# Gram stage with eight chunk places, tile-wise first loads on two queues, unread matmuls ahead of it, and another order of vector work around the first quad

## The reference

```python
# q, k, v: (1, 6016, 256); w_in: (256, 2048), w_out: (2048, 256), twice
qn = q / (np.linalg.norm(q, axis=1, keepdims=True) + 1e-06)   # norm over the 6016 tokens
kn = k / (np.linalg.norm(k, axis=1, keepdims=True) + 1e-06)
s = kn.transpose(0, 2, 1) @ qn / tau                          # 256 x 256
s = s - s.max(-1, keepdims=True)
a = np.exp(s); a /= a.sum(-1, keepdims=True) + 1e-09
x = v @ a
h = x @ w_in1;  r = np.maximum(h, 0.0);  x = (r * r) @ w_out1
h = x @ w_in2;  y = np.maximum(0.01 * h, h) @ w_out2
```

## Time and profile before

| | |
|---|---|
| median of 3 runs | 1044.88 us |
| the profiled execution | 1044.72 us, its span 1042.9 us (1.8 us lie around the span) |
| PE busy | 1025.2 us, 98% |
| DVE busy | 733.9 us, 70% |
| ACT busy | 670.3 us, 64% |
| granted TensorE clock, mean | 0.999 of full |
| DMA moved | 69.24 MB |

### The profile page before, as it was taken

The page is one execution under the profiler, slowest core; times in us unless marked ns, Lnnn a source line. Parts: engine busy times, 40 slices in busy tenths (PEclk is TensorE's granted clock), DMA queues, the critical chain, the costliest instruction groups (busy, mean ns, idle before and its releaser), DMA issues.

```text
span 1042.9 us, 13073 instructions
## 1 busy us (share of the span) xinstructions
PE 1025.2 (98%) x4596; PEld 858.9 (82%) x4596; DVE 733.9 (70%) x1176; ACT 670.3 (64%) x1155; POOL 0.8 (0%) x7
## 2 busy tenths in 40 slices
PE   7989999999999999999999999999999999999998
PEld 6868888888888888888888888888888888888886
DVE  6888866657666665766657777777777777767665
ACT  5768877767767777667676655556556555555553
POOL 0000000000000000000000000000000000000000
PEclk9999999999999999999999999999999999999999
DMA  8810111122122112205344002002002002000001
GB/s 297 317 60 21 31 50 71 66 96 70 47 94 84 53 56 100 76 29 189 120 166 155 1 1 80 1 1 79 1 1 79 0 1 80 1 1 26 14 1 41
DMA packets 33552, 69.24 MB, mean 66 GB/s; under 512 B 2768, under 2 KB 18128, under 8 KB 33488
## 3 DMA queue, kind: packets, MB, share of 16 engines
q1 hardware_dynamic: 33488, 68.43, 19.3%
HBM read 44.56 MB, written 23.86 MB: 66 GB/s over the span
## 4 chain that ended last, share of the span: by engine, by line
PE 93%; DVE 3%; DMA 1%; ACT 1%; issue 1%; SPq 0%; ACTq 0%; DVEq 0%
PE bank L443 30%; PE bank L445 30%; PE bank L444 30%; PE bank L450 2%; DMA qk<-in_k 1%; DVE sq_sum L877 1%; DVE xop_lo L911 0%; DVE raw L902 0%; DVE g L1077 0%; ACT park_down L719 0%; ACT g L770 0%; DVE wi_lo L883 0%; ACT qk_hi L640 0%; DVE qk_lo L871 0%; DVE sq_sum L887 0%
## 5 line engine op out<-in xcount | busy, mean ns | idle before, releaser
L738 ACT ACTIVATE g_hi<-g 128x496 fp32r<-128x496 f32 (+1 forms) x384 | 237.2, 618 | 214.3 <-DVE g L1031 76.4
L1021 DVE TENSOR_TENSOR g_lo<-g,g_hi 128x496 fp32r<-128x496 f32 (+1 forms) x384 | 259.9, 677 | 128.7 <-ACT g_hi L738 127.1
L445 PE MATMUL bank<-g_hi,wout_lo 128*128 128x496 f32 (+1 forms) x768 | 296.4, 386 | 0.0
L444 PE MATMUL bank<-g_lo,wout_hi 128*128 128x496 f32 (+1 forms) x768 | 296.0, 385 | 0.0
L443 PE MATMUL bank<-g_hi,wout_hi 128*128 128x496 f32 (+1 forms) x768 | 295.9, 385 | 0.0
L443 PE MATMUL bank<-xop_hi,win_hi 128*128 128x496 f32 (+1 forms) x672 | 260.2, 387 | 4.1 <-DVE win_lo L936 2.2
L444 PE MATMUL bank<-xop_lo,win_hi 128*128 128x496 f32 (+1 forms) x672 | 259.3, 386 | 0.0
L445 PE MATMUL bank<-xop_hi,win_lo 128*128 128x496 f32 (+1 forms) x672 | 259.0, 385 | 0.0
L443 PEld LDWEIGHTS bank<-g_hi,wout_hi 128*128 128x128 f32 x768 | 144.3, 188 | 27.5
L444 PEld LDWEIGHTS bank<-g_lo,wout_hi 128*128 128x128 f32 x768 | 144.3, 188 | 27.3
L445 PEld LDWEIGHTS bank<-g_hi,wout_lo 128*128 128x128 f32 x768 | 144.2, 188 | 27.0
(11 more groups left out here) (98 smaller groups left out, 665.8 us busy)
## 6 DMA issues: line engine op xcount, KB each, us to landing
up_parts<-park_up SPq DMA_DIRECT2D x8, 896.0 KB, 4.3
qk<-in_q SPq DMA_DIRECT2D x15, 384.0 KB, 4.6
qk<-in_k SPq DMA_DIRECT2D x15, 384.0 KB, 6.2
stage_o<-in_w_out SPq DMA_DIRECT2D x16, 256.0 KB, 3.4
down_parts<-park_down SPq DMA_DIRECT2D x8, 512.0 KB, 2.8
raw<-in_vT SPq DMA_DIRECT2D x8, 496.0 KB, 4.9
x_tiles<-out_buf SPq DMA_DIRECT2D x8, 496.0 KB, 2.8
raw<-x_tiles SPq DMA_DIRECT2D x8, 496.0 KB, 4.2
```

Source lines behind the costliest of these rows:

```text
L444: pe.matmul(out, a_hi, b_lo, start=False, stop=False, **more)
L445: last = pe.matmul(out, a_lo, b_hi, start=False, stop=stop and i == len(operands) - 1, **more)
L738: act.activation(g_hi[:, tile, 0:W], g[:, tile, 0:W], ACT.Copy).then_inc(g_hi_made[tile], 1)
L1021: dve.tensor_tensor(g_lo[:, tile, 0:W], g[:, tile, 0:W], g_hi[:, tile, 0:W].bitcast(F32), ALU.subtract).then_inc(g_split[tile], 1)
```

## The change

Loads: the Gram stage has eight chunk places, the loops are written out, and the first edge tile comes alone (128 KB each of q and k). Its k and the k of chunks 0 and 1 are issued from ACT's queue, the rest from SP's. The second edge tile comes ahead of chunk 3, raw0 behind the second piece of w_in1. PE does seven matmuls on a constant tile ahead of the first load; nobody reads them. The sums stand behind the first tile of the last chunk instead of ahead of it. Around the first quad the order of ACT, DVE and PE work is another, and DVE's `fold_scale_first` goes to ACT.

```diff
-QK_SLOTS = 5
+QK_SLOTS = 8
-SPLIT_SLOTS = (2,)
+SPLIT_CHUNKS = (2, 7, 12)
+EARLY_CHUNKS = 2
+WARM_UP = 7
...
+            def load_chunk(c):
+                if c >= QK_SLOTS:
+                    sp.wait_ge(chunk_used, c - QK_SLOTS + 1)
+                    sp.wait_ge(squared, squares_at(c - QK_SLOTS) + 1)
...
+            sp.dma_start(edge[:, 0, 0, :], q_t[:, 0, :]).then_inc(edge_loaded[0], 16)
+            for c in range(EARLY_CHUNKS):
+                sp.dma_start(qk[:, c, 0, :, :], q_t[:, chunk_tokens(c), :]).then_inc(qk_loaded[c], 16)
+            for c in range(EARLY_CHUNKS, QK_CHUNKS):
+                if c == EDGES_AFTER:
+                    load_edge(1)
+                load_chunk(c)
...
-                if c == 2 * QK_SLOTS - 1:
-                    load_raw0()
...
                 sp.dma_start(held, w_in1_b[:, :, n * FCOLS:(n + 1) * FCOLS]).then_inc(stage_loaded[n], 16)
+                if n == 1:
+                    load_raw0()
...
+            pe.wait_ge(constants, 1)
+            for i in range(WARM_UP):
+                pe.matmul(fold[0][:, 0:P], ones[:, :], ones[:, :], start=True, stop=True)
...
+                    if c == QK_CHUNKS - 1 and t == 0:
+                        pe.wait_ge(chunk_added, QK_CHUNKS + 1 + QK_TILES)
+                        for i in range(2):
+                            for b in range(CB):
+                                total = pe.matmul(sums[:, i, b, :], sq_sum[:, i, 0, b * P:(b + 1) * P], ones[:, 0:2],
+                                                  start=True, stop=True)
+                        total.then_inc(sums_ready, 1)
...
                 product(0, bank_a[:, 0:W], A11, B11, True).then_inc(p1_ready, 1)
-                fold_unit(4)
...
                 product(0, bank_c[:, 0:W], S1, T1, True).then_inc(p5_ready, 1)
-                fold_unit(5)
+                fold_unit(4)
...
                 product(0, bank_a[:, 0:W], A12, B21, False).then_inc(c11_ready, 1)
+                fold_unit(5)
                 fold_unit(6)
...
+            act.dma_start(edge[:, 1, 0, :], k_t[:, 0, :]).then_inc(edge_loaded[0], 16)
+            for c in range(EARLY_CHUNKS):
+                act.dma_start(qk[:, c, 1, :, :], k_t[:, bass.ds(EDGES + c * QK_TILES, QK_TILES), :]
+                              ).then_inc(qk_loaded[c], 16)
...
-            x_high(0, 0)
             weights_hi(0)
             weights_hi(1)
...
             act.activation(warm[:, 1:2], ones[:, 0:1], ACT.Exp)
+            x_high(0, 0)
             x_high(0, 1)
             weights_hi(2)
...
-                x_high(0, 2)
-                x_high(0, 3)
                 fold_scale(0, 0)
+                fold_scale(0, 1)
                 up_high(0)
...
             x_sum(0, T1)
-            weights_lo(0)
...
-            weights_lo(1)
+            weights_lo(0)
             dve.wait_ge(q_row_ready, 1)
...
+                if Q == 0:
+                    up_sums_low(1)
                 if G == 0:
                     down_low(quad)
-                if Q == 0:
-                    up_sums_low(1)
```

More of the change, by code:

```diff
@@ L151, in channel_attention_two_mlps @@
         qk = at("qk", [P, QK_SLOTS, 2, QK_TILES, C], F32, o_xh0)
[L152 to L156, removed]
+        sq_sum = at("sq_sum", [P, 2, QK_TILES, C], F32, o_xh0 + 49152)
+        edge = at("edge", [P, 2, EDGES, C], F32, o_xh0 + 55296)
+        qk_hi = at("qk_hi", [P, 2, QK_TILES, C], F32R, o_wout_hi)
+        qk_lo = at("qk_lo", [P, 2, QK_TILES, C], F32R, o_wout_hi + 6144)
         sq = at("sq", [P, SQ_SLOTS, 2, QK_TILES, C], F32, o_wout_hi + 12288)
@@ L187, in channel_attention_two_mlps @@
         assert UNITS == len(fold)
-        edge_loaded = sem("edge_loaded")
+        edge_loaded = [sem(f"edge_loaded{t}") for t in range(EDGES)]
         qk_loaded = [sem(f"qk_loaded{i}") for i in range(QK_SLOTS)]
@@ L277, in chunks_before, with squares_at @@
         def chunks_before(part, low):
-            last_byte = (7 * low + part + 1) * ROW_COLS * 4 - 1
-            return QK_CHUNKS - QK_SLOTS + min(last_byte // SLOT_BYTES, QK_SLOTS - 1) + 1
+            slot = ((7 * low + part + 1) * ROW_COLS * 4 - 1) // SLOT_BYTES
+            return max(c for c in range(QK_CHUNKS) if c % QK_SLOTS == slot) + 1
+        EDGES_AFTER = 3
+        def squares_at(c):
+            return c if c < EDGES_AFTER else c + 1
         def raw_row(G, part):
@@ L506, in _ @@
                 pe.wait_ge(exp_ready, i + 1)
+                pe.wait_ge(constants, 2)
                 for j in range(CB):
@@ L991, in park_down_low @@
                                   ALU.subtract).then_inc(down_split, 1)
-            def fold_scale_first():
-                dve.wait_ge(fold_ready, 2)
-                dve.wait_ge(e_inv_ready, 1)
-                dve.tensor_scalar(folded[0][:, :, A12:A22 + 1, :], fold[1].rearrange("p (s h c) -> p s h c", s=2, h=2),
-                                  e_inv[:, 1:2], None, ALU.mult).then_inc(fold_scaled[1], 1)
+            weights_lo(1)
+            x_low(0, 0)
+            x_low(0, 1)
+            up_add(0)
+            up_low(0)
+            up_sums_low(0)
             x_sum(0, T2)
-            x_low(0, 0)
             weights_lo(2)
-            fold_scale_first()
-            up_low(0)
-            up_add(0)
-            x_low(0, 1)
-            up_sums_low(0)
             x_low(0, 2)
+            x_low(0, 3)
             weights_lo(3)
-            x_low(0, 3)
             x_sum(0, T3)
+            x_sum(0, T4)
             x_low(0, 4)
             x_low(0, 5)
-            x_sum(0, T4)
             x_low(0, 6)
```

147 lines of the change are left out of this document (66 added, 81 removed).

## The result

The changed kernel takes **1038.24 us** (median of 4 runs, 1037.6 to 1038.34) against 1044.68 (4 runs, 1044.3 to 1045.94): ratio 0.9935, 95% interval 0.9918 to 0.9952. The forecast was 1040.5 with a range of 1038.5 to 1043.0. The direction is right; the gain is 6.4 us where 4.3 were forecast, and the time lies 0.26 us under the range.

What follows compares the result with a forecast made beforehand. PE, busy 1025.2 of 1042.9 us, bounds the kernel; the start of P5 of window 1 counts. Legs of 1.6 + 1.2 + 1.5 = 4.3 us give 1040.5 us, range 1038.5 to 1043.0 for 8 in 10.

Steps and rivals of the forecast that it cites:

- Leg 1: From the start to chunk 2 on PE, now 16.35 us: gain 1.6 us, bounds 0 and 2.6.
- the landing of chunk 0: In the first loads: chunk 0 lands at 7.6 us instead of 8.76, at the earliest 6.6.
- Edge tile 1 moved out of the way: In the first loads: 0.26 MB less ahead of chunk 0, which then lands at 7.9 us.
- The second queue: In the first loads: issuing the k of chunk 0 earlier is worth between nothing and 0.9 us, taken as 0.3.
- 0.75 MB behind a load: In the first loads: a load is reported when 0.75 MB behind it have moved, so chunk 0 lands at 1.80 MB.
- The 0.45 us for the unread matmuls: PE at chunks 0 and 1: seven unread matmuls lift the clock, worth 0.45 us and no more.
- Leg 2: From chunk 2 to exp, now 37.82 us: gain 1.2 us, bounds 0.5 and 1.8, with ACT late next.
- Leg 3: From e_inv to P5 of window 1, where DVE's list is the leg: gain 1.5 us, bounds 0 and 2.3.
- Start as before: Rival at the first loads: smaller edge load and second queue bring nothing; 3.2 us gained, 1041.7 us; chance 0.18.
- ACT bound: Rival at the first quad: ACT has two jobs more, leg 3 falls to 0; 2.8 us gained, 1042.1; chance 0.18.
- Slower by raw0: Rival ahead of the norms: raw0 lands late, x_sum holds up the softmax; 1049 us at 280 GB/s; chance 0.04.
- More than forecast: Whole kernel: landing at 6.6 us and waits gone, down to 1038 us; chance 0.1.

Runs made afterwards that it cites:

- one_queue: The changed kernel with all early loads issued by SP instead of SP and ACT: 1039.85 us, ratio 0.9955 to the kernel before.
- five_places: The changed kernel with five chunk places as before instead of eight: 1039.21 us, ratio 0.9934 to the kernel before.
- no_unread: The changed kernel without the seven matmuls whose result nobody reads: 1038.40 us, ratio 0.9939 to the kernel before.
- edge_whole: The changed kernel with both edge tiles ahead of the chunks, as one load of 2 KB rows for each queue: 1038.86 us.
- x_high_ahead: The changed kernel with ACT's first two copies of x ahead of its wait for the sums: 1037.70 us, ratio 0.9927 to the kernel before.
- sums_ahead: The changed kernel with the sums ahead of the whole last chunk, not behind its first tile: 1037.73 us, ratio 0.9934 to the kernel before.
- raw_early: The changed kernel with raw0 loaded behind chunk 9 as before: 1039.40 us, ratio 0.9950 to the kernel before.
- group 1: The follow-up runs on the start, timed in rounds with the kernel before, whose median there was 1044.84 us.
- before_two_queues: The kernel before with the k of the edges and of the first two chunks issued by ACT, nothing else changed: 1044.65 us, ratio 1.0002.
- old_quad: The changed kernel with the first quad in the order of before on PE, ACT and DVE: 1040.30 us, ratio 0.9941 to the kernel before.
- split_later: The changed kernel with chunks 7, 10 and 13 split instead of 2, 7 and 12: 1037.46 us, ratio 0.9919 to the kernel before.
- edges_first: The changed kernel with both edge tiles ahead of the chunks, as four loads on two queues: 1042.06 us, ratio 0.9974 to the kernel before.

## Why the prediction was right in direction and too small

**Leg 1, the step that failed: the landing of chunk 0.** I put it at 7.6 us, with 6.6 as the bound, and its k and q were there at 5.59. one_queue stands between my two steps. Edge tile 1 moved out of the way was to bring the landing to 7.9 on one queue; one_queue has chunk 0 at 6.28, so this step was 1.6 us too small. The second queue was to bring 0.3 us; it brings 0.7 for chunk 0 and 1.25 for chunk 2, which is what PE waits on. My bound of 0.9 was worked out for chunk 0 alone; the loads of chunk 2 are issued 1.4 us earlier. one_queue also holds the eight places and the unread matmuls, but five_places and no_unread have chunk 0 at 5.61 and 5.60 without them. The two steps do not simply add: taken the other way round, the queue is worth 2.06 us on the kernel before, and the edge tile 1.57 (edge_whole against after).

Two assumptions carried the landing. One was that 0.75 MB behind a load must have moved before it is reported. The table shows 0.28 to 1.08 MB, so this is no constant; with the rates measured after (218 GB/s to 5 us, then 404) my 1.80 MB would have landed at 6.8, so it accounts for 1.2 of the 2.0 us. The other was the rate itself, taken from before, 0.8 us. It was also read a little wrong: 324 GB/s is the mean to 10 us, up to the landing it was 309.

On the second queue the Trainium skill's "DMA: Bandwidth & Descriptors" (Issuing engines are not separate DMA queues) says that a second issuer saves only the issuing time, and calls that time usually small. With the changed order the runs bear out the first half: 0.69 us of landing for 0.95 us of earlier issue. They don't bear out that it is small here. On the kernel before they go against both: 2.06 us for 0.94, with 414 GB/s against 247 from 3.5 to 6 us, at equal bytes and with loads enough issued. Why the rate was low there these runs don't say. I had read the page as if the 0.3 us fell away by it, though they were issuing time.

Behind the landing my chain held better: 7.59 us from there to chunk 2, forecast 7.15, as chunk 1 came late (8.18) and pushed the split. The 24 records at full pace and the 1.8 us wait for the split came as said (5.47 and 1.73). The 0.45 us for the unread matmuls were wrong: without them chunk 2 starts at 13.15. I had compared PE at low pace with a landing at 7.6; in no_unread PE is on chunk 0 at 5.62 and through chunk 1 7.50 us later, just when DVE has the split ready.

**Leg 2** was forecast 36.6 us long and is 36.26. The wait for sq_sum is gone, exp starts with ACT and not DVE just ahead of it (x_high_ahead), and ACT's chain from the sums to exp takes 4.57 us where I had 4.7. (My sum to the end of the sums, 31.9, is 32.0 when added up again.) The margin was smaller than I had it: DVE's fold ends 37.3 us behind the landing, not 35.9, and DVE has 1.0 us to spare ahead of the sums, not 2. Of these, 0.9 are the new place of the sums; sums_ahead takes it away and loses nothing, with 0.2 left. What puts DVE in time is above all the load's place, which raw_early undoes for a loss of 1.2 to 1.8 us. raw0's new place was a rival for slower in my text, and no gain. DVE takes x_sum at 42.80 without waiting; at 369 GB/s from 10 to 45 us, where the earlier trace rows had 346, that rival was further off than I had it.

**Leg 3** was forecast 1.5 us and gave 1.39; the path from the end of e_inv to P5 is 18.1 us (forecast 17.9), with DVE busy 16.97 (16.9) and PE's wait for wi_lo 0.77 (1.0). The rival that ACT becomes the bound did not come: behind P5 PE waits for no copy of ACT.

**Left out: the clock behind the waits.** Nothing in the forecast priced a clock that falls in the middle of the kernel. Before has two long waits of PE (1.7 and 2.2 us), and its 19 runs of group 1 spread from 1043.3 to 1048.5 with mean clocks from 1.000 down to 0.996; after lies within 0.7 us at 0.999 to 1.000. before_two_queues and old_quad show a stretch at 0.50 behind such waits, which cost 1.4 and 1.6 us in the one and 1.2 in the other (P5 and the five records behind it: 2.73 us against 1.49). five_places shows one behind its wait for the split, 1.0 us, where after has the same wait and none. In "TensorE: Matmul & The Clock Gate" of the Trainium skill (The HAM clock gate) the clock is said to follow PE's recent activity and to vary from run to run. The rows agree in this much: the clock fell behind waits, and behind the same wait in one execution and not in another. It did not lengthen the profiled execution of before, so it is no part of the table of the legs; in the medians its share is small (the gain of the medians is 6.4 like that of the profiles) but it is what took most of the gain of before_two_queues in its profile.

**Rivals.** Start as before: wrong, it gained twice what I gave it. ACT bound: wrong. Slower by raw0: wrong in sign. More than forecast, down to 1038, which had 0.1, is where the result lies.

## What to carry to other kernels

Before a rate is taken from the old trace for a new order of loads, ask what held it there: here the first 9 us ran at 169 and 309 GB/s and with the new order at 218 and 404, so the range of a landing needs the full rate as its other end. Price an earlier issue at the load that PE waits on, not at the first one. What stood first did best here as few large loads, with what PE needs last moved behind. And where a start is made earlier, find each list that was in time by a little: here DVE's up to the sums took back half of the wait that split_later removed.

## What the runs showed of the hardware

- Of the same loads, 207 GB/s were moved in the first 5 us from two queues (before_two_queues) and 169 from one (before), then 409 against 309 until chunk 0 was squared. The difference is made between 3.5 and 6 us (414 against 247), with 1.6 MB issued and not yet moved on the one queue. With edge tile 1 later one queue also came to 403 from 5 us on, and edges_first stood at 337 with two queues: the number of queues is not all of it.
- Four loads of 1 KB rows at the head of two queues put the following load 2.3 us later (9.44) than two loads of 2 KB rows with the same bytes (7.16). The bytes moved by then were 2.39 against 1.90 MB, so loads behind it moved meanwhile. Why is open.
- The granted clock fell to 0.50 in or behind PE waits of 1.65 and 2.17 us (before_two_queues), 2.17 (old_quad) and 1.80 (five_places), and stayed at 1.00 at waits of 1.66 and 2.17 us in before, 1.73 in after and 2.45 in one_queue. The stretch at 0.50 cost 1.0 to 1.6 us.
- The 24 records of the first two chunks took 0.33 and 0.31 us each on average in before and no_unread and 0.23 in after, and the four of the first edge tile 2.08 us in before, where those of the second take 1.03. The granted clock was recorded as 1.00 in all of them: the record at the start of a trace can show 1.00 where the pace is that of the lower level.
- When the pace rises behind the same unread matmuls varies: the four records of the edge tile took 1.91 us in after and 1.03 in five_places.
